# A fused attention, expert and mixing kernel: dummy matmuls in the routing's waits, token rows stored in two steps

## What is computed

```python
scores = scale * q @ k.T + bias          # keys: the first n_global = 8, and the last n_local = 96
x = softmax(masked scores) @ v           # (B, S, D)

# expert stage: E = 8 experts, F = 1024; one expert for each token
fresh = argmax(x @ w_gate)
e[s] = fresh[s] if s == 0 or sigmoid(x[s] @ w_local) < 0.5 else e[s - 1]
x = softmax(x @ w_gate)[e] * (relu(x @ w1[e]) @ w2[e])

# mixing stage
theta = x @ w_theta
y = w_tok_r @ (x * cos(theta)) + w_tok_i @ (x * sin(theta))     # over tokens
u = x + y
out = u + relu(u @ w_ch)
```

## Time and profile before

| | us |
|---|---|
| median of 3 runs | 525.03 (524.4 to 525.05) |
| profiled execution, its own time | 525.41 |
| its span, first to last instruction | 523.6 |
| TensorE busy | 499.9 |
| VectorE busy | 271.2 |
| ScalarE busy | 199.5 |
| GpSimd busy | 108.8 |

### The profile page before, as it was taken

How to read it: one execution, slowest core, us unless ns; L and a number is a source line. 1 busy time by engine, 2 the same in 40 slices (tenths; PEclk the granted TensorE clock), 3 DMA queues, 4 the chain that set the end, 5 groups by cost and what they waited for, 6 DMA issues and landing times.

```text
span 523.6 us, 9451 instructions
## 1 busy us (share of the span) xinstructions
PE 499.9 (95%) x3416; PEld 437.1 (83%) x3416; DVE 271.2 (52%) x633; ACT 199.5 (38%) x425; POOL 108.8 (21%) x114
## 2 busy tenths in 40 slices
PE   9899999758999999999999999999999999999997
PEld 9678888548999999999899899878788878888885
DVE  4687878674115151515415411478887684455143
ACT  2988887312114141414414311445544232322010
POOL 3998680002112121212212111000000000000000
PEclk9999999959999999999999999999999999999999
DMA  8545318163925555556955500150000000000012
GB/s 335 222 132 201 129 52 334 43 242 118 385 90 214 226 213 223 223 208 240 390 226 220 230 24 20 46 200 0 1 0 1 1 1 20 21 20 21 20 61 80
DMA packets 19128, 71.15 MB, mean 136 GB/s; under 512 B 2702, under 2 KB 2702, under 8 KB 14864
## 3 DMA queue, kind: packets, MB, share of 16 engines
q1 hardware_dynamic: 16304, 63.88, 32.0%
q0 software_dynamic: 2640, 6.30, 3.4%
q10 hardware_dynamic: 144, 0.44, 0.2%
HBM read 62.49 MB, written 10.49 MB: 139 GB/s over the span
## 4 chain that ended last, share of the span: by engine, by line
PE 75%; DMA 8%; DVE 7%; ACT 4%; issue 4%; SPq 1%; POOLq 0%; DVEq 0%; ACTq 0%; POOL 0%
PE ps L1312 41%; PE ps L1341 19%; DMA w_sb<-in_w_experts 4%; PE ps L1244 3%; PE ps L1207 3%; ACT prob L646 2%; PE ps L1227 2%; PE ps L1167 2%; DMA x_rows<-x_tok 2%; PE ps L1182 2%; PE ps L1328 1%; PE ps L1413 1%; DMA x_tok<-y_rows 1%; ACT z_hi L737 1%; DMA xin<-x_rows,token_at 1%
## 5 line engine op out<-in xcount | busy, mean ns | idle before, releaser
L1341 PEld LDWEIGHTS ps<-xT,w_sb 128*128 128x128 f32 x1024 | 116.5, 192 | 3.6 <-issue 2.0
L1341 PE MATMUL ps<-xT,w_sb 128*128 128x128 f32 x1024 | 117.1, 275 | 1.6 <-DMA w_sb<-in_w_experts 1.2
L1047 DVE SCALAR_TENSOR_TENSOR hT_lo<-ps,hT_hi 128x512 fp32r<-128x512 f32 x32 | 22.1, 690 | 99.4 <-ACT hT_hi L700 99.3
L1056 DVE TENSOR_TENSOR w_lo<-w_sb,w_hi 128x1024 fp32r<-128x1024 f32 x32 | 37.1, 1221 | 39.2 <-ACT w_hi L711 39.2
L1312 PE MATMUL ps<-w_hi,hT_hi 128*128 128x512 f32 x128 | 51.2, 400 | 0.0
L646 ACT ACTIVATE prob<-raw,row_min 128x256 f32<-128x256 f32 (+1 forms) x96 | 45.9, 480 | 12.6 <-DVE row_min L893 12.5
L1312 PE MATMUL ps<-w_lo,hT_hi 128*128 128x512 f32 x128 | 49.9, 390 | 0.0
L1312 PE MATMUL ps<-w_hi,hT_lo 128*128 128x512 f32 x128 | 49.9, 390 | 0.0
L700 ACT ACTIVATE hT_hi<-ps 128x512 fp32r<-128x512 f32 x32 | 19.1, 597 | 74.5 <-PE ps L1341 74.5
L704 ACT COPY yout<-ps 128x512 f32<-128x512 f32 x16 | 9.4, 587 | 84.8 <-PE ps L1312 84.8
L711 ACT CAST w_hi<-w_sb 128x1024 fp32r<-128x1024 f32 x32 | 31.1, 1043 | 12.6 <-DVE first_tile L1032 12.5
(11 more groups left out here) (173 smaller groups left out, 944.4 us busy)
## 6 DMA issues: line engine op xcount, KB each, us to landing
w_sb<-in_w_experts SPq DMA_DIRECT2D x32, 1024.0 KB
v_sb<-in_vx SPq DMA_DIRECT2D x8, 640.0 KB, 4.1
q_raw<-in_q SPq DMA_DIRECT2D x8, 384.0 KB, 5.8
x_rows<-x_tok SPq DMA_DIRECT2D x2, 1536.0 KB, 7.8
x_tok<-y_rows SPq DMA_DIRECT2D x12, 256.0 KB, 5.2
out_x<-o_sb SPq DMA_DIRECT2D x12, 256.0 KB, 2.0
k_raw<-in_kx SPq DMA_DIRECT2D x7, 432.0 KB, 4.8
wtr<-in_w_tok_rT SPq DMA_DIRECT2D x6, 384.0 KB
```

Source lines behind the costliest of these rows:

```text
L1047: dve.scalar_tensor_tensor(hT_lo[:, part, :], ps[:, 1 + half, :].rearrange("p (c q) -> p c q", c=4), 0.0, hT_hi[:, part, :].bitcast(F32), ...
L1056: dve.tensor_tensor(quarter(w_lo, par, q), quarter(w_sb, par, q), w2_hi_quarter(q).bitcast(F32), ALU.subtract).then_inc(s_w2_lo, 1)
L1341: last = pe.matmul(ps[:, 1 + half, f * P:(f + 1) * P], w_sb[:, par, c // 2, j:j + P], xT[:, c, :], start=(c == 0), stop=(c == DC - 1))
```

## The change

Dummy matmuls go into four places of TensorE's list: 10 before it waits for the routing's first value, 3 and 3 before the next two waits, and 20 before it waits for `in_tile`. And SyncE stores x_rows in two steps: the columns of heads 0 to 5 (1536 B of each row) once 12 pieces of x_tok are there, and those of heads 6 and 7 (512 B of each row) once all 16 are; GpSimd's wait counts four DMAs in place of two.

```diff
-            sp.wait_ge(s_x_done, PAIRS // GROUP)
-            for b in range(B):
-                sp.dma_start(x_rows.rearrange("(b i p) d -> b p i d", b=B, p=P)[b],
-                             x_tok[:, b * QT:(b + 1) * QT, :]).then_inc(s_x_out, 16)
+            for first, last in ((0, H - 2), (H - 2, H)):
+                cols = slice(first * DH, last * DH)
+                sp.wait_ge(s_x_done, 2 * last)
+                for b in range(B):
+                    sp.dma_start(x_rows.rearrange("(b i p) d -> b p i d", b=B, p=P)[b, :, :, cols],
+                                 x_tok[:, b * QT:(b + 1) * QT, cols]).then_inc(s_x_out, 16)
...
-            pool.wait_ge(s_x_out, 16 * B)
+            pool.wait_ge(s_x_out, 2 * 16 * B)
...
+            keep_running(10, 4)
             pe.wait_ge(s_p_ready, 1)
             pe.matmul(ps[0:NT, 5, 0:P], gate_m[:, 3, :], ident, start=True, stop=True).then_inc(s_row_mm, 1)
+            keep_running(3, 4)
             pe.wait_ge(s_row_d, 1)
             pe.matmul(ps[0:NT, 6, 0:NT], con("before")[0:NT, 0:NT], ends[:, 0, :], start=True,
                       stop=True).then_inc(s_row_mm, 1)
+            keep_running(3, 4)
             pe.wait_ge(s_row_d, 2)
...
+            keep_running(20, 4)
             pe.wait_ge(s_in_tile, 1)
```

## The result

| | kernel before | changed kernel |
|---|---|---|
| median, us | 524.98 (12 runs, 523.45 to 526.01) | 527.14 (12 runs, 525.84 to 529.55) |
| ratio to before, 95% interval | | 1.0049 [1.0035, 1.0064] |
| profiled execution: span, us | 523.6 | 525.9 |
| its mean granted clock | 0.987 | 0.997 |

The changed kernel is slower by 0.35 to 0.64%, some 2.2 us by the medians, although in the profiled execution TensorE has the full clock in all of the routing now. The profiled execution took 527.81 us, 0.7 us above the median.

What follows compares the result with a forecast made beforehand. Bound: busy TensorE, with expert work set by routing and store releasing the gather. Ten dummies +2.23, clock −0.5, the store's 0.33 taken off: gather +1.40 us, so 525.03 + 1.4 = 526.4 us; range 523.9 to 528.5.

Steps and rivals of the forecast that it cites:

- the prediction's own signs of being wrong: Dummies filling 101.6 to 103.8, 1.2 GHz behind 104.3, or 122.42 to the end changing by more than a few tenths.
- The ten dummies wait for a page: After the attention: dummies start only with TensorE's code at 104.3 and hold L1295 back by 2.23 us.
- The clock in the routing: TensorE's full clock stays through the routing and gives back 0.5 us, bounded by zero and 0.9.
- the first rival: The clock falls all the same; if during the ten dummies, 526.8 to 528.8 us; chance 0.13.
- The twenty: Before in_tile: 4.47 us of dummies make L1320 about 0.9 us late, but it catches up; cost zero.
- The margin of the store: Before the gather: the x_rows store is last by only 0.33 us, all that moving it gives by itself.
- Nothing behind the gather: Matmuls at 120.89 and 122.42 ran at full clock already, so nothing is won there.

Runs made afterwards that it cites:

- the reordered forms: Kernel before with TensorE's two attention forms in the other order (whole_rows in the If, windows in the Else): 532.21 us, ratio 1.014.
- the routing moved ahead of the jump: TensorE's routing written into both attention forms: changed kernel, 4 dummies behind the jump for 11, 525.12 us; kernel with the two-step store, no routing dummies, 527.69 us.
- 19: Changed kernel with 19 instead of 11 dummies behind L1320's counterpart, up to the gathered rows: 526.83 us, ratio 1.0038.
- 15: Changed kernel with 15 instead of 11 dummies behind L1320's counterpart: 526.85 us, ratio 1.0032.
- five: Changed kernel with five first dummies instead of ten: 527.12 us, ratio 1.0045.
- the ten alone: Kernel before with only the ten dummies ahead of L1295, store still in one step: 528.31 us (4 runs), ratio 1.006.
- seven: Kernel before with the two-step store and seven dummies ahead of the wait for in_tile: 523.45 us, ratio 0.9977.

## Why the prediction was right, and where it was not

The time lay in the range and on the side forecast: 527.14 us against 526.4, a change of 2.2 us against 1.4. But of the prediction's own signs of being wrong one came up: the stretch from the first expert tile to the end, 401.2 us before, is 402.5 us (123.43 to 525.9), 1.3 us more and not a few tenths. By its wording a second one did too: the clock rows show 1.2 GHz behind 104.3, though not in the routing. Point by point:

**The ten dummies wait for a page.** Right, and shown by the jump's own record (3.85 us), by the reordered forms and by the routing moved ahead of the jump. The first dummy was expected near 104.3 and came at 104.30. From the page on they cost 2.43 us (104.30 to 106.73) where the kernel before took 0.06; but the page came at the same time in both executions and `gate_m` 0.29 us later in this one, so behind `gate_m` the delay is 2.10 us, against 2.23. That the two agree so well is chance.

**The clock in the routing.** Right in the profiled execution: from L1295 to the end of `token_at` it is 11.08 us instead of 11.51, so 0.43 us against 0.5. But the chance of 0.13 for the first rival, a fall during the dummies, was far too low: of five traces with dummies right behind that jump (the changed kernel, 19, 15, five, and the ten alone) four show it, between 103.3 and 105.1. With 15 and 19 the fall put L1298 3.6 to 3.7 us behind `gate_m` instead of 2.8.

**The twenty.** Right for the full clock: L1326 started at 115.12, about 1 us late, and followed `at_place` to its end.

**The margin of the store.** The failed term of the sum. The prediction let GpSimd take 0.9 us after whichever came last. It takes 0.88 us after the row of the store's landing, and 0.30 after `token_at`. So the store had been the last by 0.9 us and not 0.33 (the second step itself landed 4.4 us behind its piece of x_tok, forecast at 5 to 6, and was off the chain), and the sum up to the gather is 2.10 − 0.43 − 0.91 = +0.76 (measured +0.75), not +1.40.

**Nothing behind the gather.** The failed step. It was put down as "The matmuls that follow at 120.89 and 122.42 ran at full clock already, so nothing is won there": true, but it did not ask what is lost. The eleven dummies had lasted until 120.0 only because most of them ran at half clock. Their end at full clock was to be had from the earlier trace rows and the prediction's own terms: they would start 2.23 − 0.5 us later than 115.48, at 117.2, and end 11 x 0.223 us later, at 119.7, with the rows due at 120.84 + 1.40 = 122.2. That is an idle time of 2.5 us (measured 1.75) which needed a price. In the profiled execution the full clock was lost behind it, on the first expert tile: +1.52 us. The trace with five first dummies has the same idle time without the fall, so +1.52 is what it cost here and not in every execution.

The two errors, −0.65 and +1.5, have opposite signs. The mechanism of the ten is shown; that the total came within 0.8 us owes something to chance.

## What to carry to other kernels

Before dummies are put into an idle stretch, see why it is idle: if the engine has no code there, because a jump has just been made, they start when the real work could have, and delay it by their length. A count of dummies is sized in time, and its time halves when the clock doubles: every group behind a place where the clock is regained must be counted anew, or the fall can come where the real work starts. And where two things release a step at nearly the same time, the difference of their rows is not the margin: compare the step's start behind the one and behind the other.

## What the runs showed of the hardware

A jump of TensorE to code that is not there took 3.41 to 3.85 us at the end of the attention in nine traces and 3.94 us with ten dummies ahead of it, 3.46 and 3.47 us where it was moved behind the routing, and 6.08 us at the start of the attention. The Trainium skill, "Runtime: NRT & Kernel Launch", section "Instruction fetch mechanics", has the rule (the target page is loaded by DMA before the engine can go on), and these runs agree with it. The durations are measured here. TensorE's instruction packet started about 1 us behind the start of the jump's record at the end of the attention (100.4 to 101.4 in the kernel before) and behind the routing, 1.5 us behind it with ten dummies ahead of the jump (101.3 to 102.8), and 3.5 us behind it at the start (10.5 to 14.0). So work that TensorE still has ahead of a jump can put off the page; what exactly the packet waits for isn't shown.

ScalarE's wait for its page behind the same block was 2.12 to 2.29 us in the three traces with the store in one step, and 3.24 to 4.16 us in the ten with the two-step store, whose first step was in the rings at that time (until 102.0 in the changed kernel). It was off the path. That the store's packets are what holds up the page is an inference; no trace shows it directly. The row of the changed kernel:

```profile
103.06 0.40 ACT L694 CAST exact_c<-cst 128x256 fp32r<-128x256 f32 x1 [3.84 <-issue]
```

Packets of 512 B nearly follow their bytes too. The hardware queue of the changed kernel from 109.5 to 112.7 us (packets, MB, share of 16 engines):

```profile
q1 hardware_dynamic: 1568, 0.79, 81.1%
```

That is 81.1% x 16 x 3.2 us / 1536 = 27 ns for one, 0.053 ns per byte against the 0.0434 of 2048 B packets, and the second step landed 4.4 us behind its piece of x_tok.

In three traces the clock fell behind the twelve 20-column matmuls of the map, although TensorE's records show hardly a gap there: at 118.46 with 19 dummies, 118.74 with 15 and 115.09 with seven. In the changed kernel and with five first dummies the same twelve stand in the same place, and the clock stayed full behind them. What decides is open.
